# Slot weighting of three batches inside the last MLP, and a causal mask added to the decay rows

## The reference

```python
def _attn_ref(q, k, v, f):          # 4 batches, 8 heads, 576 tokens, width 64
    ...
    scores = scale * np.matmul(q, k.transpose(0, 1, 3, 2))
    log_f = np.log(np.clip(f, 0.0001, 1.0))
    cum = np.cumsum(log_f, axis=-1)
    decay = cum[:, :, :, None] - cum[:, :, None, :]
    causal = np.triu(np.ones((S, S), dtype=bool), k=1)
    scores = np.where(causal, -1000000000.0, scores + decay)
    ...
    return np.matmul(attn, v).astype(np.float32)      # attn: softmax over the keys

def _moe_ref(x, w_in, w_out):       # 2304 tokens, 512 to 2048 to 512
    h = x @ w_in
    g = h * (1.0 / (1.0 + np.exp(-1.702 * h)))
    return (g @ w_out).astype(np.float32)

def _moe2_ref(x, phi, w1, w2):      # 8 experts of 4 slots, 512 to 1024 to 512
    logits = x @ phi
    d = logits - logits.max(0, keepdims=True)
    d = np.exp(d)
    d /= d.sum(0, keepdims=True) + 1e-09
    slot_input = d.T @ x
    ...
        h = np.maximum(slot_input[e] @ w1[e], 0.0)
        slot_out[e] = h @ w2[e]
    ...
    return (c @ slot_out).astype(np.float32)          # c: softmax of logits over the slots
```

## Time and profile before

| | us |
|---|---|
| median of 3 runs | 764.37 (763.54 to 765.16) |
| the profiled execution | 765.94 |
| its span, first to last instruction | 764.2 |
| PE busy in the span | 717.7 |
| attention beside MLPs 0 to 2 | about 110 to 560 |
| MLP 3 alone | about 570 to 687 |
| slot softmax and summing | 687 to 703 |
| experts | 703 to 746 |
| mixing and writing | 746 to 764 |

### The profile page before, as it was taken

How to read it: one execution, slowest core, us unless ns; L and a number is a source line. 1 busy time by engine, 2 the same in 40 slices (tenths; PEclk the granted TensorE clock), 3 DMA queues, 4 the chain that set the end, 5 groups by cost and what they waited for, 6 DMA issues and landing times.

```text
span 764.2 us, 15776 instructions
## 1 busy us (share of the span) xinstructions
PE 717.7 (94%) x6027; PEld 681.0 (89%) x6027; DVE 444.7 (58%) x1255; ACT 437.0 (57%) x1031; POOL 399.3 (52%) x439
## 2 busy tenths in 40 slices
PE   3999979999999999999999999999999999998993
PEld 3888879999999999999999989999999999995562
DVE  5898957676776646675656466766542332224323
ACT  4788866575757675666576665757554344311113
POOL 4355357474747764565657564848385476520000
PEclk9999989999999999999999999999999999998897
DMA  4433323332333333333331413332214454598976
GB/s 104 106 92 106 94 65 89 87 94 81 95 94 96 95 94 81 87 105 91 100 91 51 126 28 95 94 108 67 69 43 141 135 169 163 161 401 348 357 307 247
DMA packets 90362, 96.65 MB, mean 126 GB/s; under 512 B 61296, under 2 KB 61296, under 8 KB 88240
## 3 DMA queue, kind: packets, MB, share of 16 engines
q1 hardware_dynamic: 90288, 95.66, 40.6%
HBM read 90.84 MB, written 4.79 MB: 125 GB/s over the span
## 4 chain that ended last, share of the span: by engine, by line
PE 79%; DVE 10%; ACT 7%; issue 2%; DMA 0%; POOL 0%; SPq 0%; DVEq 0%; POOLq 0%
PE mb L1204 51%; PE yb L1057 6%; PE zb L1076 6%; PE xb L1103 5%; PE mb L1256 2%; DVE prob L838 2%; PE xb L1037 2%; ACT prob L689 2%; PE yb L1295 1%; ACT xh L713 1%; DVE ptl L844 1%; PE yb L1059 1%; DVE kl L806 1%; DVE qs L802 1%; ACT qs L681 1%
## 5 line engine op out<-in xcount | busy, mean ns | idle before, releaser
L1204 PE MATMUL mb<-xh,wih 128*128 128x288 f32 x512 | 159.1, 311 | 7.8 <-DVE xl L855 4.3
L1204 PE MATMUL mb<-gh,woh 128*128 128x288 f32 x512 | 156.5, 306 | 3.5 <-DVE x2t L932 3.5
L1204 PE MATMUL mb<-xl,wih 128*128 128x288 f32 x512 | 151.6, 296 | 0.0
L1204 PE MATMUL mb<-xh,wil 128*128 128x288 f32 x512 | 151.6, 296 | 0.0
L1204 PE MATMUL mb<-gl,woh 128*128 128x288 f32 x512 | 150.8, 294 | 0.0
L1204 PE MATMUL mb<-gh,wol 128*128 128x288 f32 x512 | 150.8, 294 | 0.0
L643 POOL TENSOR_TENSOR gl<-hid,gh 128x288 fp32r<-128x288 f32 x128 | 105.0, 825 | 74.9 <-ACT gh L730 73.3
L925 DVE SCALAR_TENSOR_TENSOR hid<-gate,mb 128x288 f32<-128x288 f32 x128 | 57.7, 451 | 116.0 <-ACT gate L736 114.9
L689 ACT ACTIVATE prob<-prob,m_row 64x576 f32<-64x576 f32 (+4 forms) x160 | 96.4, 604 | 35.3 <-DVE m_row L824 34.4
L660 POOL TENSOR_TENSOR wol<-stage,woh 128x512 fp32r<-128x512 f32 x64 | 82.9, 1295 | 62.0 <-ACT woh L675 62.0
L660 POOL TENSOR_TENSOR wil<-stage,wih 128x512 fp32r<-128x512 f32 x64 | 82.1, 1290 | 57.0 <-ACT wih L675 56.9
(11 more groups left out here) (196 smaller groups left out, 1471.1 us busy)
## 6 DMA issues: line engine op xcount, KB each, us to landing
stage<-in_moe_w_in SPq DMA_DIRECT2D x64, 256.0 KB, 3.0
stage<-in_moe_w_out SPq DMA_DIRECT2D x64, 256.0 KB, 2.6
ring_a<-in_moe_w SPq DMA_DIRECT2D x16, 1024.0 KB, 6.9
ring_b<-in_moe_w SPq DMA_DIRECT2D x14, 1024.0 KB, 11.8
cum_b<-cum_dram SPq DMA_DIRECT2D x32, 288.0 KB, 3.7
qk_in<-in_q SPq DMA_DIRECT2D x32, 144.0 KB, 3.0
qk_in<-in_k SPq DMA_DIRECT2D x32, 144.0 KB, 3.5
v_in<-in_v SPq DMA_DIRECT2D x32, 128.0 KB, 3.2
```

Of the source, the lines that this page charges most:

```text
L1204: ins = mm(bank[:, 0:HALF], a[:, t, P * (j % 4):P * (j % 4) + P], x[:, t, cols], start=(i == 0), stop=(i == 11))
```

## The change

**The mask.** From batch 1 on (24 of 32 heads) no mask matmul is issued. SP loads five copies of the head's row instead of one, of 576, 512, 384, 128 and 256 columns, one for each query tile, into `cum_t`: a buffer of 1920 columns, for odd heads where `cum_b` was, for even heads in the part of `x2tok` that batch 2's tokens will fill later. A new GpSimd step "cmask", ahead of "dup", adds `mask` to the diagonal blocks of all five in two instructions (3 blocks of 128 columns and 2 blocks). DVE's L824 reads this in place of `cum_b`.

```diff
+                for i in (4, 3, 2, 0, 1):
+                    w = P * i + QW[i]
+                    sp.dma_start(cum_t[s % 2][:, COFF[i]:COFF[i] + w], cum_dram[bass.ds(n, 1), 0:w].to_broadcast([P, w])
+                                 ).then_inc(c_dma[s % 2], 16)
...
+                elif st[0] == "cmask":
...
+                    pool.wait_ge(c_dma[n % 2], cum_loaded(n))
+                    c = cum_t[n % 2]
+                    for at in (c[:, P * 4:CW].rearrange("p (x n) -> p x n", n=P)[:, 0:11:5, :],
+                               c[:, P * 3:P * 12].rearrange("p (x n) -> p x n", n=P)[:, 0:5:4, :]):
+                        pool.tensor_tensor(at, at, mask[:, :].unsqueeze(1).broadcast_to([P, at.shape[1], P]), ALU.add
+                                           ).then_inc(c_masked, 1)
...
-                        ins = mm(ybf[:, base + P * i:base + P * i + r], ident_r[:, :], mask_r[:, 0:r],
-                                 start=False, stop=True, skip_group_check=True)
...
+                        if b == 0:
+                            ins = mm(ybf[:, base + P * i:base + P * i + r], ident_r[:, :], mask_r[:, 0:r],
+                                     start=False, stop=True, skip_group_check=True)
```

```diff
-BUSY = (9, 3, 14)
+BUSY = (4, 2, 8, 5)
+EARLY = 3 * QT
+EARLY_AT = {"maxima": 10, "turn_max": 12, "max": 13, "spread": 15, "weigh": 16, "exp": 17, "sums": 19,
+            "send0": 20, "send1": 21, "send2": 22, "send3": 23, "total": 24, "keep": 26}
...
+    return (held_steps(m) + mlp_steps(m, 0, U_MLP - 2) + [(0, ("post", 0))] + mlp_steps(m, U_MLP - 2, U_MLP - 1)
+            + [(0, ("post", 1))] + mlp_steps(m, U_MLP - 1, U_MLP) + [(0, ("post", 2))])
```

```diff
+                elif st == ("post", 0):
+                    nc.vector.memset(last_logits[32:64, P:P + 64], -3e38)
+                    nc.vector.memset(last_logits[64:P, P:P + 64], -3e38).then_inc(edge_made, 1)
+                elif st == ("post", 2):
+                    dve.wait_ge(post_logits, m + 2)
+                    nc.vector.tensor_reduce(bmax[:, :], last_logits[:, 0:P + 64], AX_X, ALU.max).then_inc(max_raw, 1)
...
+            nc.vector.scalar_tensor_tensor(out=acc[:, :], in0=acc[:, :], scalar=kept[:, 0:1], in1=last_sent,
+                                           op0=ALU.mult, op1=ALU.add).then_inc(acc_made, 1)
...
+                elif st == ("post", 0):
+                    pe.wait_ge(unit_out, m * U_MLP + U_MLP + 2 - 4)
+                    pe.wait_ge(edge_made, 1)
```

```diff
-                    if last and j == 2:
+                    if last and u % 2 and u // 8 < len(ring_a):
                         sp.wait_ge(x_lo, 4 * BATCH)
-                        load_half_expert(u // 16, u % 16 // 8)
+                        load_expert_part(u // 8, u // 2 % 4, 4)
+                    at = u - RING_X_AT
+                    if last and at >= 0 and at % 2 == 0 and at // 8 < len(ring_x):
+                        sp.wait_ge(acc_made, 1)
+                        load_expert_part(len(ring_a) + at // 8, at // 2 % 4, 4)
```

More of the change, by code:

```diff
@@ L42 @@
 PW = 1920
+CW = 1920
+COFF = [512, 1024, 640, 0, 1280]
 PT_ALL = 1600
@@ L109, in mlp_steps @@
             steps.append((-1, ("turn", 0)))
+        if m == BATCH - 1:
+            steps += [(0, ("early", kind)) for kind in EARLY_AT if EARLY_AT[kind] == u]
     return steps
@@ L188, in batch_steps @@
         if engine == "pool":
-            qk, dup = qk + dup, []
+            qk, dup = following_head("cmask") + qk + dup, []
         norm = at(scoring, "norm", s)
@@ L497, in load_w, with load_expert_part @@
                 sp.dma_start(stage[:, slot, :], src).then_inc(w_dma[slot], 16)
-            def load_half_expert(e, half):
+            def load_expert_part(e, part, parts):
                 w = (w1[e // 2].rearrange("(p t) n -> p t n", t=KM) if e % 2 == 0
@@ L966, in _ @@
[L966 to L973 removed]
+            m = BATCH - 1
@@ L1140, in slot_logits @@
+            def slot_logits(bank, tiles, t0, t1):
+                for t in range(t0, t1):
                     for i in tiles:
@@ L1246, in _ @@
-            pe.wait_ge(t_dve, 10)
+            m = BATCH - 1
+            pe.wait_ge(max_made, 2)
+            tr(top_row[0:1, 0:P], low_max[:, 1:2], ident[:, :]).then_inc(top_turned, 1)
+            busy(BUSY[0], last_sent)
+            pe.wait_ge(e_made, 1)
+            turn_slots(last_turn, et).then_inc(e_turned, 1)
+            pe.wait_ge(row_made, 2)
+            mm(top_back[:, 0:1], row[:, :, :].rearrange("o g s -> o (g s)"), ident[0:1, 0:1], start=True, stop=True
+               ).then_inc(top_spread, 1)
@@ new lines, in _ @@
+            busy(BUSY[1], last_sent)
+            pe.wait_ge(ewt_made, 1)
+            pe.wait_ge(token_out, 1 + QT * BATCH)
+            for i in range(QT):
+                g, r = i % 4, QW[i]
+                if i == 4:
+                    pe.wait_ge(den_in, 1)
+                    mm(top_row[:, 0:1], blk4[:, :, :].rearrange("p g s -> p (g s)"), part_sum[:, :], start=True, stop=True
+                       ).then_inc(den_made, 1)
+                ins = mm(last_sent[32 * g:32 * g + SLOTS, :], ewt[0:r, i, :], x2last[0:r, i, :],
+                         start=(i < 4), stop=(i > 0), skip_group_check=True)
@@ L1248, in up, with loaded @@
+            busy(BUSY[3], top_back)
+            pe.wait_ge(slot_made, 1)
+            def loaded(a):
+                pe.wait_ge(e_dma[a % NR], 16 * sum(4 if x < len(ring_a) + len(ring_x) else 2 for x in range(a % NR, a + 1, NR)))
             def up(e):
                 a = 2 * e
-                pe.wait_ge(e_dma[a % NR], 32 * (a // NR + 1))
+                loaded(a)
                 if e >= 2:
```

454 lines of the change are left out of this document (304 added, 150 removed).

## The result

The changed kernel takes 840.16 us (838.23 to 843.99, 4 runs) where the kernel before takes 764.76 beside it (4 runs): ratio 1.0988 (95% interval 1.0958 to 1.1018). It is ten per cent slower; the forecast was 1.3% faster, and the rival on the decay rows, which ends on this side, had said 771. The profiled execution took 841.07 us with a span of 839.1.

What follows compares the result with a forecast made beforehand. PE's instruction stream was taken as the bound in attention, MLPs and experts, a latency chain in the tail. From the median 764.37 us, -12.3 + 2 + 1.5 + 3.7 + 1 - 5.9 = -10.0 gave 754.4 us, range 747 to 761.

Steps and rivals of the forecast that it cites:

- the rival on the decay rows: Attention: five rows land much later than one did, cmask and copies of k end late, PE waits; 771 us, chance 0.08.
- Step 2, the landing: Attention heads: five decay rows, 950 KB, take some 7 us to move; up to 0.5 us more lost in tight heads.
- Step 2, the price of lateness: PE's waits for late copies of k: +2 us (0 to 6), heads 8 and 9 +1.5; some 20 at 9 us landings.
- Step 2, GpSimd's time: cmask takes GpSimd 1.75 us a head, 42 us in all; the engine idles 175 of 450 us, so only place matters.
- Step 1, the mask matmuls: Attention on PE: 22 heads x 5 removed mask matmuls at 0.112 us each, heads 8 and 9 uncounted; -12.3 us.
- Steps 3 to 5: Last MLP and tail: work moved into the MLP, expert quarters ahead of weights, shorter tail; +3.7, +1 and -5.9 us.
- step 3: Last MLP: 30 passes put into gapless PE cost 3.4 us, five small instructions 0.3; together +3.7 us.
- step 4: Last MLP: 512 KB quarters of experts queued ahead of the tight fourth weight piece, five groups; +1 us (0 to 5).
- step 5: Tail: first `up` 8.6 us behind the last unit, 7.4 less; transposes and a drain given back earlier; net -5.9 us.
- The drain of ("post", 0): Near the last MLP's end: PE sits idle some 0.8 us waiting for `edge_made`, which DVE sets behind unit 61's eviction.
- the rival on the clock in the tail: Tail: the shorter chain with fillers keeps PE's clock up, winning 3.6 us and part of the summing matmuls; 750.3, chance 0.15.
- the ring: DMA behind the last MLP: 20 MB instead of 24 MB to come, experts stay bound by PE; counted as nothing.

Runs made afterwards that it cites:

- e1: The changed kernel with its mask part undone (one decay row a head, mask matmuls in all heads, no cmask), tail and ring as changed: 767.49 us, ratio 1.0046.
- e6: e1 without the mask matmuls of batches 1 to 3 and no mask in their place, so scores there are not causal: 757.90 us, ratio 0.9923.
- e7: e1 plus cmask's two GpSimd instructions a head ahead of the copies of k, on a buffer nothing reads: 776.54 us, ratio 1.0165.
- e5: The changed kernel with its five loads kept and read by DVE, mask added on PE as before, no cmask: 769.17 us, ratio 1.0055.
- e10: The changed kernel, five loads and all, with cmask behind the two copies of k on GpSimd instead of ahead: 773.53 us, ratio 1.0132.
- e4: The changed kernel with each partition's five loads reading a DRAM row of its own, from a weight array, so other decay data: 785.13 us, ratio 1.0280.
- e12: e1 with experts loaded as before, 1 MB every eighth unit, and the two added ring places filled behind the last unit: 766.24 us, ratio 1.0034.
- e3: The changed kernel with one load of 1856 columns a head, from a table laid out once in DRAM, replacing the five: 770.69 us, ratio 1.0087.

## Why the prediction was wrong

The parts as measured, in medians: tail part +3.2 (e1), matmuls -9.6 (e6), cmask +9.0 (e7), loads +1.7 (e5). They add up to 768.6 in the changed kernel. It took 840.2. The 71.6 us that are left belong to none of the parts; they are what cmask and the late loads make together, and the order "cmask ahead of the copies" is what joins them (e10 takes 66.6 of them away). Their size can be read in the pages of the changed kernel and e5. PE's waits ahead of L1230 are 62.6 against 7.6 us, 55.0 more. PE is busy 734.8 us against 717.9, though it lacks the matmuls that are 13.3 us of busy time between e1 and e6 (718.8 and 705.5): 30.2 us more, the low clock behind the waits. 55.0 + 30.2 - 13.3 = 71.9 of the 73.8 us between the two spans. The clock rows say nearly the same: from 80 us to the last MLP PE is busy 59.8 us at the low level in the changed kernel and 6.1 in e5, and half of the difference, by estimate what it costs, is 27 us.

**Step 2, the landing, failed.** I took 7 us from the first issue to the last landing, from one row's 3.7 us and the weights' rate. The last one landed 10.9 us behind it in the mean of 24 heads and cmask started 11.5 us behind it, 13.0 and 13.1 in head 21. The rival had the mechanism whole, the same place, the same chain and even its reason (all partitions read one row of DRAM), and I gave it 0.08. The argument against it was the queue at 87 GB/s and a share of 0.32. That is a mean over bytes, and this cost does not go by bytes: in the changed kernel the share is 0.44 at 101 GB/s. Nor could have told: one decay row of 288 KB lands after 3.7 us, but in e4 the first of the five, from rows of its own, takes 3.8 and 3.9. The price shows from the second load on, 1.5 to 1.9 us for each, so five loads were to be counted as five and not as 950 KB; only a kernel with several such loads in a row shows it.

**Step 2, the price of lateness, failed too.** For landings of 9 us I had waits of 20 us. At 10.9 in the mean they are 55, and the low clock adds 27 to 30, which stands nowhere in the prediction. I had looked at the clock in the tail only; the earlier trace rows shows it full through the attention stage, where PE idles 8.6 of 450 us. In the changed kernel it idles 59 of 540, and the clock falls behind the waits.

**Step 2, GpSimd's time.** The two instructions took 1.67 to 1.99 us, mostly 1.7, where I had 1.75, and cost 9.0 us instead of 3.5. What failed is that, of 42 us on an engine that idles 175 of 450, "load is no matter": some of DVE's instructions stand still while GpSimd runs, so part of GpSimd's idle time was DVE's running time. The trace of before held it. There, as in e1, 14 of the 128 rescalings take 0.90 to 1.51 us, each with a GpSimd instruction beside it, where the others mostly take 0.29 to 0.48.

**Step 1, the mask matmuls:** right in kind and in the price of one, 9.6 instead of 12.3 us in all. PE's busy time ahead of the last MLP fell by 0.106 us a matmul (e6) where I had 0.11; what is missing is what comes behind it, PE's idle time there, which grew by 2.5 us, mostly for evictions of the units. And two heads' matmuls, which I had left out, are in it. The Trainium skill ("TensorE: Matmul & The Clock Gate", Back-to-back issue gap) has some 81 ns for such a matmul; the net 0.080 us of e6 come out at that figure, but PE's busy time does not, so the agreement is chance as far as these runs show.

**Steps 3 to 5, into the last MLP and the tail:** forecast 3.7 + 1 - 5.9 = -1.2, measured +3.2 (e1) and +2.1 without the quarters (e12). By the traces the last MLP became 8.5 us longer in e1 (from 108.0 to 116.5) where step 3, step 4 and the give-backs of step 5 had 6.2. From start to start the 30 passes take 4.0 us and not 3.4: one costs 0.13 us between units where 40 in a row cost 0.11 each. The small early steps take 0.9 us where I had 0.3, the transposes 0.6, the drain 1.0 and e12's wait 0.5; and the matmuls of the units themselves take 1.6 us more with other work between them, for which I had nothing. The drain of ("post", 0) was right, 0.96 us of idle against 0.8:

```profile
761.29 1.07 PE L1357 MATMUL yb<-x2t,phi_sb 128*32 128x128 f32 x16 [0.96 <-DVE x2t L1100]
```

Behind the last unit the chain that ended last reads so in the changed kernel, against the earlier trace rows:

```profile
765.64 1.60 PE mb L1421 x12
774.46 1.85 PE xb L1456 x8
777.44 3.57 PE mb L1473 x32
782.17 1.99 PE mb L1473 x32
```

The first `up` starts 10.1 us behind the end of the last unit (777.37 - 767.24; 9.6 in e1) where I had 8.6 and the kernel before 16.0; it is at the low clock as before, the second nearly at the full one, so the rival on the clock in the tail came true in part: the low stretch there is 6.8 us long instead of 10.2. From the end of the last unit to the end of the span, ten traces with the changed tail give 69.3 to 71.9 us, mean 70.9, and four with the old one 75.6 to 78.4, mean 77.1: a gain of 6.2 there, 8.5 given for it in the MLP. Moving work out of a latency chain into a stretch where PE is the bound pays only if the chain becomes shorter by more than the work costs PE there.

**Right:** no wait of PE for `wil` or `wol`, the ring at nothing, and the sentence at the end: wrong above all if PE waits in every head for k.

## What to carry to other kernels

Ahead of an engine's in-order queue, ask of each wait that you add what stands behind it; a wait that costs next to nothing at the end of a step can be the dearest ahead of it (66.6 us for one line). Two changes that are cheap alone, a late load (1.7 us) and a short step in front of a copy (9.0 us), are to be priced together: here they cost 71.6 us on top. GpSimd's idle time is not free where DVE is busy, and a stall of some us in a stretch where PE runs at full clock cost about one and a half times its length here.

## What the runs showed of the hardware

- Of five loads in a row that each give one DRAM row to 128 partitions, each landed 1.5 to 1.9 us behind the one ahead of it (means of 24 heads), 64 KB (1.75) like 256 KB (1.70); the first of the five, 288 KB, was no slower than from separate rows (3.8 and 4.0 us in the changed kernel, 3.8 and 3.9 in e4). In head 21 cmask could start 13.1 us behind the first issue of five such loads; five of the same sizes from separate rows had landed after 7.6 us (e4), one of 928 KB after 7.4 us (e3).
- DVE's addition to 5 columns took 0.97 us and its rescaling 0.9 to 1.6 us while GpSimd instructions ran, where rescalings mostly take 0.29 to 0.48 us; the fused decay step and the evictions kept their times (means of 536 to 539 and 451 to 455 ns in all kernels).
- Behind PE's wait of 7.27 us the granted clock was 0.50 for the 4 us shown; over the changed kernel such stretches cost 27 to 30 us more than in e5, by estimate.
